# Second-layer attention: the products with the values for two pairs at a time

## What is computed

```python
for e in range(4):
    q, k, v = x @ wq[e], x @ wk[e], x @ wv[e]            # (768, 64)
    scores = where(causal, -1e9, q @ k.T / 8)
    a = exp(scores - scores.max(-1)); a /= a.sum(-1) + 1e-9
    ye = a @ v @ wo[e]
    out += (mixing weight of e where e is among the two best) * ye
```

## Time and profile before

| | us |
|---|---|
| median of three runs (lowest, highest) | 477.29 (473.89, 477.82) |
| the profiled execution | 476.8 |
| its span | 475.1 |
| matmuls busy (TensorE) | 429.8 |
| weight loads busy (TensorE, beside the matmuls) | 385.3 |
| VectorE busy | 286.6 |
| ScalarE busy | 211.7 |
| GpSimd busy | 116.0 |

### The profile page before, as it was taken

One profiled execution on the slowest core, in us unless ns is written; L12 is line 12 of the kernel. 1 busy time (PEld: TensorE's weight loads), 2 busy tenths in 40 slices (PEclk: granted clock), 3 DMA queues, 4 the chain that ended last, 5 costly groups with the idle time before them and its releaser, 6 DMA issues.

```text
span 475.1 us, 9670 instructions
## 1 busy us (share of the span) xinstructions
PE 429.8 (90%) x3108; PEld 385.3 (81%) x3109; DVE 286.6 (60%) x629; ACT 211.7 (45%) x415; POOL 116.0 (24%) x126
## 2 busy tenths in 40 slices
PE   3799999943999999999999999849989999999987
PEld 2788888833989898989898989649977779987775
DVE  3499999975555555555555656433687642477750
ACT  1123223251445454545464545414476644466653
POOL 0646465420110101010100000063049710015330
PEclk9999999985899999999999999959999999999999
DMA  7976657317768777676766684154220003220003
GB/s 235 311 255 209 209 176 237 139 68 281 257 215 294 257 253 248 244 251 241 256 230 221 221 285 157 38 146 127 69 65 2 1 24 112 61 71 0 0 0 132
DMA packets 32723, 78.37 MB, mean 165 GB/s; under 512 B 4032, under 2 KB 4160, under 8 KB 32704
## 3 DMA queue, kind: packets, MB, share of 16 engines
q1 hardware_dynamic: 25888, 58.21, 37.2%
q0 software_dynamic: 4512, 15.73, 9.7%
q10 hardware_dynamic: 2304, 4.20, 2.3%
HBM read 57.67 MB, written 17.30 MB: 158 GB/s over the span
## 4 chain that ended last, share of the span: by engine, by line
PE 76%; DVE 9%; issue 6%; DMA 5%; ACT 2%; SPq 1%; POOL 1%; DVEq 0%; ACTq 0%; POOLq 0%
PE bank L1189 7%; PE bank L1191 7%; PE bank L1190 7%; PE bank L1206 6%; PE bank L1204 6%; PE bank L1205 6%; PE bank L1308 5%; PE bank L1293 4%; PE bank L1275 3%; PE bank L1279 2%; PE bank L1251 2%; PE bank L1250 2%; PE bank L1249 2%; PE bank L1169 2%; DMA dec<-in_decay 2%
## 5 line engine op out<-in xcount | busy, mean ns | idle before, releaser
L1189 PE MATMUL bank<-xh,w1h 128*128 128x256 f32 x256 | 73.8, 288 | 0.9 <-DVE xl L905 0.9
L1191 PE MATMUL bank<-xh,w1l 128*128 128x256 f32 x256 | 73.6, 288 | 0.0
L1190 PE MATMUL bank<-xl,w1h 128*128 128x256 f32 x256 | 73.6, 288 | 0.0
L899 DVE TENSOR_TENSOR w2l<-raw,w2h 128x1024 fp32r<-128x1024 f32 x32 | 37.1, 1222 | 42.5 <-ACT w2h L583 42.5
L520 POOL TENSOR_SCALAR att<-att,stat,mixw 128x128 f32<-128x128 f32 (+5 forms) x48 | 34.0, 718 | 89.5 <-DVE stat L1038 89.5
L583 ACT ACTIVATE w2h<-raw 128x1024 fp32r<-128x1024 f32 x32 | 31.7, 1050 | 47.5 <-PE bank L1206 45.5
L1189 PEld LDWEIGHTS bank<-xh,w1h 128*128 128x128 f32 x256 | 50.5, 197 | 1.3 <-DVE xl L905 1.0
L1190 PEld LDWEIGHTS bank<-xl,w1h 128*128 128x128 f32 x256 | 50.4, 197 | 0.3
L1204 PE MATMUL bank<-w2h,hh 128*128 128x512 f32 x128 | 50.6, 395 | 0.0
L1191 PEld LDWEIGHTS bank<-xh,w1l 128*128 128x128 f32 x256 | 50.4, 197 | 0.0
L1206 PE MATMUL bank<-w2h,hl 128*128 128x512 f32 x128 | 49.9, 390 | 0.0
(11 more groups left out here) (158 smaller groups left out, 974.6 us busy)
## 6 DMA issues: line engine op xcount, KB each, us to landing
raw<-in_w SPq DMA_DIRECT2D x64, 512.0 KB, 5.9
xr<-tokens_by_expert POOLq DMA_DIRECT2D x8, 512.0 KB, 4.0
outputs_by_expert<-ysb ACTq DMA_DIRECT2D x16, 256.0 KB, 6.1
tokens_by_expert<-zero POOLq DMA_DIRECT2D x7, 512.0 KB, 6.2
q_in<-in_qT SPq DMA_DIRECT2D x12, 256.0 KB, 2.8
kz_in<-in_kT SPq DMA_DIRECT2D x24, 128.0 KB, 3.8
k_in<-in_kR SPq DMA_DIRECT2D x12, 256.0 KB, 3.8
v_in<-in_vR SPq DMA_DIRECT2D x12, 256.0 KB, 4.3
```

The source lines that it names most:

```text
L899: dve.tensor_tensor(part(low), raw[:, q, :], part(high).bitcast(F32), ALU.subtract).then_inc(w_lo, 1)
L1189: pe.matmul(to, w1h[:, dc, at], xh[:, dc, :], start=(dc == 0), stop=False)
L1190: pe.matmul(to, w1h[:, dc, at], xl[:, dc, :], start=False, stop=False)
L1191: last = pe.matmul(to, w1l[:, dc, at], xh[:, dc, :], start=False, stop=(dc == DC - 1))
```

## The change

In TensorE's loop the visits with m = 2, 6, 10, ... lose their products, and those with m = 4, 8, ..., 24 do the pair that was left out and then their own. Six visits with two pairs each take the place of twelve with one pair. The odd pairs keep their place; the even pairs 0, 2, ..., 10 come two iterations later. Nothing else is changed: the products, their waits and the orders of the other engines are as before.

```diff
-                    if m >= 2 and m % 2 == 0:
+                    if m >= 4 and m % 4 == 0:
+                        weighted_values(m // 2 - 2)
                         weighted_values(m // 2 - 1)
```

## The result

| | before | after |
|---|---|---|
| median of 20 runs (lowest, highest), us | 475.27 (472.5, 478.39) | 478.77 (476.46, 482.98) |
| profiled execution, us | 476.8 | 478.78 |
| its span, us | 475.1 | 477.1 |

The ratio is 1.0091, with a 95% interval from 1.007 to 1.0112: the kernel is slower, by 3.3 to 5.3 us. Forecast were 480.0 us, 3.2 us above the profiled execution (476.8) and 2.7 us above the first three runs' median (477.29). The profiled execution lies 1.5 us above the median of the 20 runs; so the time itself came out 1.2 us lower than forecast, while the slowdown, 3.50 us between the medians, is 0.3 us larger.

What follows compares the result with a forecast made beforehand. TensorE was taken as the bound, but narrowly. Shifts followed through one element's attention loop end at +1.6 us; two elements give 476.8 + 2 x 1.6 = 480.0 us, range 476.0 to 482.5.

Steps and rivals of the forecast that it cites:

- step 4: Unit 12's turning waits for VectorE's copy of unit 11: -0.44 us; then 20 records more put scores 17 at +0.66.
- step 1: First merge, at unit 4: the 0.7 us low-part stall goes into the wait for GpSimd; scores 9 at +0.05 us.
- (2): Scores 11 newly wait 0.4 to 0.5 us for unit 9's exponentials, yet start 0.45 us earlier than before.
- (3): Turning unit 8 hangs on the copy of unit 7, still -0.45 us; 12 records more put unit 10 at +0.21.
- (5): Scores 21 need unit 19's exponentials, late through the row maxima that follow scores 17: +0.56 us.
- (6): Scores 23 wait for exponentials as scores 11 do, +0.06 us; unit 20, hanging on unit 19's copy, also +0.06.
- (7): The tail: unit 22 +0.72 us, rows out 0 +0.47; pair 10 then stands alone on the path, rows out 1 +1.6.
- The price of a visit: On TensorE, each visit costs 0.31 us whatever it holds; six fewer per element take 3.7 us away in both.
- A: Rival: TensorE's own work sets the pace throughout, new waits do not appear; 473.1 us, chance 0.10.
- B: Rival: only the tail costs, earlier merges keep their gain; +0.6 us per element, 478.1 us; chance 0.25 together with D.
- C: Rival: long visits starve ScalarE, VectorE and GpSimd; +3.0 us per element, 482.8 us; chance 0.15.
- D: Rival: savings and new waits cancel, within 1 us of 476.8; chance 0.25 together with B.

## Why the prediction was right, point by point

The slowdown was right in sign and in size, and but for small terms in each step; in step 4 two small errors cancelled. Starts on TensorE in us after scores 4 of the second element:

| | before | after | shift | predicted |
|---|---|---|---|---|
| scores 9 (step 1) | 6.62 | 6.77 | +0.15 | +0.05 |
| scores 11 (2) | 10.03 | 9.69 | -0.34 | -0.45 |
| unit 8 (3) | 12.32 | 11.97 | -0.35 | -0.45 |
| unit 10 (3) | 15.56 | 15.87 | +0.31 | +0.21 |
| unit 12 (4) | 19.62 | 19.17 | -0.45 | -0.44 |
| scores 17 (4) | 21.31 | 21.96 | +0.65 | +0.66 |
| scores 21 (5) | 25.98 | 26.52 | +0.54 | +0.56 |
| scores 23 (6) | 29.39 | 29.44 | +0.05 | +0.06 |
| unit 20 (6) | 31.76 | 31.81 | +0.05 | +0.06 |
| unit 22 (7) | 34.58 | 35.29 | +0.71 | +0.72 |
| rows out 0 (7) | 37.26 | 37.71 | +0.45 | +0.47 |
| rows out 1 (7) | 40.28 | 41.85 | +1.57 | +1.6 |

**Step 1** was mis-sized by 0.1 us. The stall for L1004 went, and unit 4 now waits 1.06 us for GpSimd, somewhat more than the 0.8 us named. Of the 0.10 us, 0.02 are a slip in the sum: unit 4 0.15 us earlier and 0.22 us of records more make +0.07, not +0.05. Unit 4 came at 5.50 instead of 5.46, and from there to scores 9 it took 1.27 us where the terms give 1.01 + 0.22 = 1.23. The error runs through steps 2 and 3.

**Step 4** hit its -0.44 us partly by luck. Unit 10 was 0.10 us later than forecast, and the low part on VectorE with it:

```profile
442.34 0.69 DVE L1054 TENSOR_TENSOR avl<-bank,avh 128x512 fp32r<-128x512 f32 x1 [0.20 <-ACT avh L702]
442.95 0.42 DVE L1030 TENSOR_REDUCE stat<-bank 128x1 f32<-128x256 f32 x1
443.28 0.55 DVE L1048 COPY attT<-bank 128x384 f32<-128x384 f32 x1
```

It ends at 443.03, 18.23 us after scores 4, where the prediction has 18.14 (442.54). But the row maximum starts at 442.95, 0.08 us before that end, and the prediction had it start at the end. So the copy stands where it was forecast (18.48), and unit 12 is at -0.45. The chain that the step names is the one that sets the time.

**Steps 2, 4 and 7** named waits that the trace before doesn't have, or has smaller, and they are there: L1275 for L684 twice, L1293 for L1048 of 0.77 us ahead of unit 12 (0.28 before), L1324 for L1054 in the tail. Those of the scores show as 0.25 rather than 0.5 us; the starts say what they cost. One sign did not come: the busy time of L1308's matmuls is 21.0 us instead of 23.6 for the same 336 records. The row of a visit holds 0.22 us beside 0.055 us for each record (0.88 us for 12 records, 1.75 for 28), and there are twelve visits fewer.

**The first element** was taken to be like the second. It is 0.29 us worse, through the scaling on GpSimd ahead of unit 11. The prediction had this as a bound of 0.3 us and cost it at nothing; that was the wrong end. With 0.3 us the sum would have been 3.5 us instead of 3.2; the two lengths give 3.43, the medians 3.50.

**The price of a visit**, 0.31 us, was 0.08 us too high at the one place where it was measured by itself, 0.23 us. It carried little of the forecast; it set rivals A and B. The seam at nothing was right.

**The rivals.** A, TensorE's work sets the pace, is refuted by the start of scores 11, 9.69 us after scores 4 where A needs about 9.1 (433.5), and by the single merges, of which none gains 0.31 us. It was also the outcome by the rule of the Trainium skill, TensorEngine Tiling (Array Packing), Tiling Modes, Key Properties: the change does halve the number of mode switches, and the gaps shrink from 3.7 to 2.1 us, so the trace agrees with the rule. What the rule is worth to the end of the kernel the measurement decides, and in this change nothing of it arrived. B, only the tail costs, has the way from unit 20 to rows out 1 right (1.5 us; measured 1.57 - 0.05 = 1.52), but unit 20 is at +0.05 us, not at -0.9: the merges ahead of it gain nothing on balance. C, starved engines, did not appear: scores 11 and unit 12 keep their minus signs (-0.34 and -0.45), and scores 23 are back at +0.05. D, no effect, is ruled out by the interval, 3.3 to 5.3 us.

## What to carry to other kernels

Work of an engine that bounds the kernel is worth more as cover for the next wait than as part of a long piece: before merging two visits, look at which wait each of them fills, and read the engine's starts, not its idle time. A visit costs 0.23 us where TensorE alone sets the pace, but at most 0.10 us of it was gained by any merge that was run alone, and the others lost, because a wait grew by more. The deferral that cost 0.9% when put behind the turning became a gain of 0.4 to 0.6% when nine pairs were put ahead of it and the tail was left as it was.

## What was not expected of the hardware

- The idle time shown ahead of a matmul can understate the stall, at the one place measured by 0.24 us: rows out 0 started 0.58 us late where 0.34 us were shown as idle, and scores 11 and 23 showed 0.25 us where 0.4 to 0.5 were forecast from the starts.
- The price of going in and out of the 128*64 tile was 0.23 us for one visit more between products of 512 columns, though the two gaps in the weight loads alone sum to 0.34 us. The matmuls themselves show no idle time at these gaps.
